# A new instruction order on all engines in the second attention pass of a three-stage kernel

## The chip, the core and the metric

The kernel runs on one core of a Trainium2 chip. The time is that of one execution on the device, in microseconds (us).

## What is computed

Three stages follow one another. The first is a linear attention with a decaying state, for 4 batches of 8 heads, 768 positions and 40 features:

```python
state = np.zeros((B, H, D, D))
for t in range(S):
    kt, vt, rt = (k[:, :, t], v[:, :, t], r[:, :, t])
    wt, at, bt = (w[:, :, t], a[:, :, t], b[:, :, t])
    y[:, :, t] = np.einsum('bhd,bhde->bhe', rt, state)
    Sa = np.einsum('bhde,bhe->bhd', state, at)
    state_decay = state * wt[:, :, None, :] - np.einsum('bhd,bhe->bhde', Sa, bt)
    state = state_decay + np.einsum('bhd,bhe->bhde', vt, kt)
```

The other two are a mixture of 8 experts over the 3072 resulting rows and a dense layer pair. The change touches the attention alone.

## The kernel before, in words

The attention takes the sequence in chunks of 64 positions. There are 24 steps (`STEPS`): 12 chunks for each half of the heads, 16 heads a step. A **first pass** (0 to about 140 us) works out what needs no state: for each step the 64x64 triangular matrix whose inverse couples the positions of a chunk. VectorE inverts two groups of four steps, GpSimd (POOL) the other four groups, and POOL's last inversion ends at 301.6 us, in the second pass. The **second pass** (about 145 to 385 us) carries the state `swt` through the 24 steps. It is what this text is about.

In a step of the second pass TensorE runs 17 batches of 16 small float32 matmuls, each of which is two instructions in the trace (x32). Each batch fills one PSUM bank (`BA` to `BD`), and `done=` names the semaphore `pe_...` (`did[...]`) that it raises. ScalarE or VectorE evicts the bank and raises `ev_...` (`out_of[...]`), for which a later batch waits (`arrive`). All orders are written by hand, one program for each engine. The names:

- `w`, `s`, `ktm`, `u`: batches 2 to 5 of a step, evicted by ScalarE. The trace shows them by operands: `bank<-vtm,g`, `bank<-eye,swt`, `bank<-eye,second`, `bank<-w_tm,inv`.
- `from_s(eye)` (`bank<-eye,st`) and `from_k(vtm)` (`bank<-vtm,ktm`) open the new state in `BD`. They need `ev_s` and `ev_ktm`.
- `z` (`bank<-sa_tm,off`): VectorE adds it to `w_tm`, for which `sa` (the second `bank<-w_tm,inv`) waits.
- `m1` (`bank<-rr,vt`): VectorE masks it (`m<-bank,later`).
- `sa`, `sat`: evicted by ScalarE. `st` closes the new state, and VectorE scales it into `swt`.
- `m2`, `g2` are masked by VectorE. `picks` (`bank<-pick,yt`) works on the rows of the step before. `y` (`bank<-m,btm`) is the last batch, and VectorE's `y_out` (two products into `yt`) evicts its bank `BB` at the start of the next step, before batch 3 (`s`) writes `BB` again.

VectorE also prepares inputs for coming steps. `suffixes(j)` scans `t_in` backward into `suf`, `prefixes(j)` takes a reciprocal and scans forward into `wq`, and `scaled(j)` makes `second` and `alpha`. `gates_of(k)` reduces `picks`' bank into `logit` and needs ScalarE's `rows_of(k)` (`picked<-bank`). On ScalarE `prepare(k)` copies step k's inverses into `inv`. For the first eight steps (`JOINED`) it first patches them with four small copies (line 705).

SyncE's queue (SP) issues nearly all loads, in program order, each behind its waits: `t_in` (776 KB, three slots), `rr`, `vt`, `vtm`, `inv_in`, and `wqx`, the half of `wq` that crosses between partitions. ScalarE issues `ax`, the crossed half of `alpha`. Where a line says L771 it is the helper `heads`, so batches are told apart by operands.

Of the kernel before, what the change touches and what calls it, by code (L numbers as in the profile page):

```python
# [18 lines left out]
C = 64  # L19
# [140 lines left out]
def attention(nc, inp, dram, keep):  # L160

    with ExitStack() as ctx:
# [10 lines left out]
        wqx = ring("wqx", 2, [PARTS, HP, WIDE])  # L173
# [21 lines left out]
        def late_part(n, **sizes):  # L195
# [37 lines left out]
        s_wqx, s_inv_in, s_g1st = ([m_.sem(f"{n}{s}") for s in two] for n in ("s_wqx", "s_inv_in", "s_g1st"))  # L233
# [14 lines left out]
        s_ready, s_choice, s_one = (m_.sem(n) for n in ("s_ready", "s_choice", "s_one"))  # L248
# [21 lines left out]
        def _(sp):  # L270
            def load_t(j):
                if j >= TR:
                    if j - TR < STEPS:
                        sp.wait_ge(s_alpha1, j - TR + 1)
                    elif j - TR == STEPS:
                        sp.wait_ge(s_alpha0, 1)
                    else:
                        sp.wait_ge(s_alpha, j - TR - STEPS)
# [47 lines left out]
            def load_rr(k):  # L326
                if k >= 1:
                    sp.wait_ge(did["m2"], k)
                sp.dma_start(rr[:, :, :], inp["rr"][k]).then_inc(s_vt_rr, 16)

            def load_vtm(k):
                if k >= 1:
                    sp.wait_ge(did["z"], k)
                sp.dma_start(vtm[:, :, :], inp["vtm"][k]).then_inc(s_ax_vtm, 16)
# [70 lines left out]
        def _(dve):  # L405
            dve.memset(keep.ones[:, :], 1.0).then_inc(s_ones, 1)
            dve.memset(keep.eye[:, :], 0.0).then_inc(s_ones, 1)
            dve.memset(restart[:, :, :], 0.0).then_inc(s_set, 1)
            dve.wait_ge(s_set, 1)
            dve.memset(restart[:, :, WIDE - 1:WIDE], 1.0).then_inc(s_set, 1)  # L410
# [5 lines left out]
            dve.wait_ge(s_set, 2)  # L416
# [21 lines left out]
            def prefixes(j):  # L438
                dve.wait_ge(s_suf, j + 1)
                dve.reciprocal(restart[:, :, 0:1], suf[j % 2][:, :, 1:2]).then_inc(s_rw, 1)  # L440
                dve.wait_ge(s_rw, j + 1)
                dve.tensor_tensor_scan(out=forward(wq[j % 3][:, :, :]), data0=forward(w_of(j)), data1=forward(restart[:, :, :]), initial=0.0,
                                       op0=ALU.mult, op1=ALU.add).then_inc(s_wq, 1)
                dve.wait_ge(s_wq, j + 1)
                if j >= STEPS:
                    dve.tensor_copy(wq[j % 3][:, :, WIDE - 1:WIDE], suf[j % 2][:, :, 1:2]).then_inc(s_wc, 1)

            def scaled(j, sem):
                dve.tensor_tensor(second[:, :, :], in_of(j, 1), suf[j % 2][:, :, 2:WIDE], ALU.mult).then_inc(s_second, 1)
                dve.tensor_tensor(alpha[:, :, :], in_of(j, 0), wq[j % 3][:, :, 0:C], ALU.mult).then_inc(sem, 1)  # L450

            def y_out(k):
                dve.wait_ge(did["y"], k + 1)
                dve.wait_ge(s_wqx[k % 2], 32 * turn(k))
                for h, scale in ((0, wq[(STEPS + k) % 3]), (1, wqx[k % 2])):
# [42 lines left out]
            scaled(STEPS, s_alpha0)  # L498
            suffixes(STEPS + 1)
            dve.wait_ge(did["g2"], 1)  # L500
            masked(g2, BC).then_inc(out_of["g2"], 1)
            prefixes(STEPS + 1)
            for k in range(STEPS):
                more = k + 1 < STEPS
                if k >= 1:
                    y_out(k - 1)
                    if k >= 2:
                        gates_of(k - 2)
                    else:
                        dve.sem_inc(out_of["pick"], 1)  # L510
                if k + 2 < STEPS:
                    suffixes(STEPS + k + 2)
                if more:
                    dve.wait_ge(did["ktm"], k + 1)
                    scaled(STEPS + k + 1, s_alpha)
                else:
                    dve.sem_inc(s_alpha, 1)
# [3 lines left out]
                dve.wait_ge(did["m1"], k + 1)  # L521
                masked(m1, BB).then_inc(out_of["m1"], 1)
                if k + 2 < STEPS:
                    prefixes(STEPS + k + 2)
                elif k + 2 == STEPS:
                    dve.wait_ge(s_iota, 8)
                    choices_top(FIRST, chain(dve, s_choice))
                else:
                    dve.memset(one_hot[:, :, FINAL], 0.0)
                    choices_one(FIRST, chain(dve, s_one)).then_inc(s_hot, 1)  # L530
# [3 lines left out]
                else:  # L534
                    dve.wait_ge(s_wqx[(k + 1) % 2], 32 * turn(k + 1))
                    for h, scale in ((0, wq[(STEPS + k + 1) % 3]), (1, wqx[(k + 1) % 2])):
# [10 lines left out]
            link = chain(dve, s_v)  # L547
# [93 lines left out]
        def _(act):  # L641
# [72 lines left out]
            def off_diagonal(k):  # L714
                act.copy(off[:, :, B:C], off_all[:, k])
# [776 lines left out]
```

## Time and profile before

| | |
|---|---|
| median of 3 runs | 1080.39 us (1077.92 to 1081.74) |
| the profiled execution's own time | 1083.37 us |
| its span in the trace | 1081.6 us |
| TensorE busy over the span | 974.9 us (90%) |
| VectorE, ScalarE, POOL busy | 605.9, 316.1, 285.7 us |
| in the second pass, 234.47 to 310.50 us | TensorE 71.43, VectorE 67.46, ScalarE 42.77, POOL 60.69 us busy of 76.03 |
| the same stretch | granted clock 1.00, DMA engines 0.87 busy, 254 GB/s |
| the pass's beginning, 150 to 172 us | granted clock 0.50 |

Busy times of different engines overlap, and a busy share says nothing of which wait ends last. A batch's start in the timeline is when its first matmul starts. "PE" is TensorE, "DVE" VectorE, "ACT" ScalarE, "POOL" GpSimd, and "SPq" is SyncE's DMA queue.

### The profile page before, as it was taken

To read this page: it belongs to the slowest core of one execution; us is meant where nothing else is said; L and a number is where in the kernel's file an instruction comes from. 1 tells how busy PE (TensorE), PEld (TensorE's weight loads), DVE (VectorE), ACT (ScalarE), POOL (GpSimd) and SP (SyncE) were. 2 spreads that over 40 slices of the span, in tenths; PEclk is the share of its full clock that TensorE was granted. 3 is DMA by queue.
4 is the path that set the end of the run, shared out by engine and by line. 5 is a ranking of instruction groups with operands and counts; after the bars stand their busy time and mean duration, and the time that the engine had idled before them with its cause. 6 is when DMAs were issued, how large, how long until landed. Compare 5 with 4: busy or idle time off the path is not lost. (4 is left out here: it accounts for less than half of the span.)

```text
span 1081.6 us, 47466 instructions
## 1 busy us (share of the span) xinstructions
PE 974.9 (90%) x21177; PEld 853.5 (79%) x21178; DVE 605.9 (56%) x981; ACT 316.1 (29%) x737; POOL 285.7 (26%) x351
## 2 busy tenths in 40 slices
PE   3425879999999998999999999979999999999997
PEld 3425769889888866888878888848999999999997
DVE  8896957898988761111211111146656565655655
ACT  5434645655555500011010010031121222222211
POOL 1008989798910003116611100051101000000000
PEclk9999977999999989999999999999999999999999
DMA  6877656998888537996884544320010101010100
GB/s 230 227 176 213 212 162 196 248 262 254 255 248 260 159 116 252 318 307 216 249 274 160 163 160 162 117 79 25 25 25 25 25 1 25 1 25 2 25 1 25
DMA packets 119984, 159.61 MB, mean 148 GB/s; under 512 B 60164, under 2 KB 91028, under 8 KB 119540
## 3 DMA queue, kind: packets, MB, share of 16 engines
q1 hardware_dynamic: 105636, 125.12, 38.5%
q0 software_dynamic: 5824, 25.28, 7.8%
q10 hardware_dynamic: 8464, 8.43, 2.4%
q8 instruction: 36, 0.59, 0.2%
q14 instruction: 24, 0.20, 0.1%
HBM read 133.15 MB, written 19.23 MB: 141 GB/s over the span
## 5 line engine op out<-in xcount | busy, mean ns | idle before, releaser
L1102 DVE TENSOR_SCALAR ht<-h_bank 128x512 f32<-128x512 f32 x62 | 42.8, 691 | 233.4 <-PE h_bank L1079 233.3
L1365 ACT CAST g_hi<-g 128x512 fp32r<-128x512 f32 x96 | 59.6, 620 | 278.6 <-DVE g L1319 278.6
L1090 PE MATMUL y_bank<-w_all,ht 128*128 x496 | 140.4, 437 | 0.3 <-DVE ht L1102 0.3
L1090 PEld LDWEIGHTS y_bank<-w_all,ht 128*128 128x128 f32 x496 | 92.7, 192 | 35.6 <-issue 1.9
L1234 PE MATMUL y_bank<-w_out_hi,g_hi 128*128 128x320 f32 x380 | 118.0, 311 | 1.4 <-DVE g_lo L1299 1.4
L1079 PE MATMUL h_bank<-xt,w 128*128 128x128 f32 x992 | 119.0, 278 | 0.0
L1234 PE MATMUL y_bank<-w_out_hi,g_lo 128*128 128x320 f32 x380 | 117.5, 309 | 0.0
L1234 PE MATMUL y_bank<-w_out_lo,g_hi 128*128 128x320 f32 x380 | 117.3, 309 | 0.0
L1079 PEld LDWEIGHTS h_bank<-xt,w 128*128 128x128 f32 x992 | 113.1, 192 | 3.8
L1221 PE MATMUL h_bank<-xt_hi,w_in_hi 128*128 128x512 f32 x288 | 113.8, 395 | 0.5 <-DVE xt_hi L1282 0.5
L1221 PE MATMUL h_bank<-xt_hi,w_in_lo 128*128 128x512 f32 x288 | 112.6, 391 | 0.0
L1315 DVE TENSOR_SCALAR neg<-h_bank,slope 128x512 f32<-128x512 f32 x96 | 72.0, 750 | 67.1 <-PE h_bank L1221 66.9
L1299 DVE TENSOR_TENSOR g_lo<-g,g_hi 128x512 fp32r<-128x512 f32 x96 | 66.5, 693 | 65.9 <-ACT g_hi L1365 65.9
L127 POOL TENSOR_TENSOR solved<-solved,share 128x31 f32<-128x31 f32 (+15 forms) x124 | 98.3, 793 | 9.7
L771 PE MATMUL bank<-alpha,second 40*64 40x64 f32 x1568 | 45.4, 271 | 59.0 <-DVE alpha L450 57.5
L124 POOL TENSOR_TENSOR share<-solved,blk 128x31 f32<-128x31 f32 (+15 forms) x124 | 91.2, 736 | 9.7
L771 PEld LDWEIGHTS bank<-alpha,second 40*64 40x64 f32 x1568 | 39.2, 180 | 62.0 <-issue 62.0
L95 POOL DMA_INDIRECT x<-x_rows_mid,order x31 | 30.2, 974 | 178.1 <-DVE order L596 101.4
L1234 PEld LDWEIGHTS y_bank<-w_out_hi,g_hi 128*128 128x128 f32 x380 | 71.4, 188 | 6.4 <-DVE g_lo L1299 2.3
L1221 PE MATMUL h_bank<-xt_lo,w_in_hi 128*128 128x512 f32 x192 | 75.3, 392 | 0.0
L1234 PEld LDWEIGHTS y_bank<-w_out_lo,g_hi 128*128 128x128 f32 x380 | 71.4, 188 | 3.1
L1183 POOL DMA_INDIRECT x<-expert_out_mid,position x24 | 25.4, 1057 | 179.4 <-POOLq L979 91.6
(207 smaller groups left out, 1763.4 us busy)
## 6 DMA issues: line engine op xcount, KB each, us to landing
w<-w_in SPq DMA_DIRECT2D x31, 1024.0 KB, 5.9
t_in<-wab_in SPq DMA_DIRECT2D x24, 776.0 KB, 6.2
t_in<-wak_in SPq DMA_DIRECT2D x24, 776.0 KB, 6.7
w_all<-w_in POOLq DMA_DIRECT2D x8, 1280.0 KB, 8.9
rr<-rr_in SPq DMA_DIRECT2D x24, 384.0 KB, 3.3
w_rest<-w_in SPq DMA_DIRECT2D x62, 128.0 KB, 3.1
vt<-vt_in SPq DMA_DIRECT2D x24, 256.0 KB, 3.9
vtm<-vtm_in SPq DMA_DIRECT2D x24, 240.0 KB, 3.4
```

What stands on the lines that cost most here:

```text
L95: pool.indirect_dma_start(out=keep.x[tile % XRING][:, 0:FEAT], out_offset=None, in_=dram["x_rows"], in_offset=bass.IndirectOffsetOnAxis(ap ...
L124: link(eng.tensor_tensor(part, q[:, 0:j + 1, j:j + 1].to_broadcast(shape), h[:, j:j + 1, j + 1:B].to_broadcast(shape), ALU.mult))
L127: link(eng.tensor_tensor(rest, rest, part, ALU.subtract))
L771: last = pe.matmul(out[HALF * to:HALF * to + rows_out, row, n * i:n * i + n], lhs, rhs, start=opens and i == 0, stop=closes and i == HP - 1)
L1079: last = pe.matmul(h_bank[s][h][:, f * ET:(f + 1) * ET], w1[s][:, k, (FH * h + f) * PARTS:(FH * h + f + 1) * PARTS], xt[s][:, k, :], start ...
L1090: last = pe.matmul(y_bank[s][:, 0:FEAT], ht[s][:, f, :], w2[:, ds(e * W2 + f * FEAT, FEAT)], start=f == 0, stop=f == NF - 1)
L1102: dve.tensor_scalar(ht[s][:, FH * n:FH * n + FH, :].rearrange("q f t -> q (f t)"), h_bank[s][n][:, :], 0.0, None, ALU.max).then_inc(s_relu, 1)
L1221: last = pe.matmul(h_bank[j % 2][:, :], w[:, k, f * PARTS:(f + 1) * PARTS], x_part[b % 2][:, k, :], start=n == 0, stop=n == len(passes) - 1)
L1234: last = pe.matmul(y_bank[n][:, 0:FEAT], g_part[j % RING][:, n * PARTS:(n + 1) * PARTS], v[:, f, :], start=f == 0 and p == 0, stop=f == NF ...
L1299: dve.tensor_tensor(g_lo[j % RING][:, :], g[j % 2][:, :], g_hi[j % RING][:, :].bitcast(F32), ALU.subtract).then_inc(s_glo, 1)
L1315: dve.tensor_scalar(neg[j % 2][:, :], h_bank[j % 2][:, :], 0.0, keep.slope[:, f:f + 1], ALU.min, ALU.mult).then_inc(s_neg, 1)
L1365: act.copy(g_hi[j % RING][:, :], g[j % 2][:, :]).then_inc(s_ghi, 1)
```

## The change

On TensorE `m1` moves from behind `z` to right behind `u`, `from_k(vtm)` from ahead of `z` to behind it, and the batch `from_k(m1)` from late in the step to ahead of `sa`. `low_part` (`z`) now reads 64 rows instead of 32. On VectorE `gates_of` goes ahead of `y_out`, `scaled` is split: `alpha` stays early, `second` goes behind the prefix scan, and `m1`'s mask goes ahead of `z`'s sum. The copy of the total into `wq` moves to ScalarE. On ScalarE half of the `off` copy comes early and the other half last. `wqx` gets a third slot. SP's order is new, and `rr` is loaded in two parts.

```diff
@@ SyncE: the loads of a step
             def load_rr(k):
-                if k >= 1:
-                    sp.wait_ge(did["m2"], k)
-                sp.dma_start(rr[:, :, :], inp["rr"][k]).then_inc(s_vt_rr, 16)
+                for part, last in ((slice(HS, HS + HP), "st"), (slice(0, HS), "m2")):
+                    if k >= 1:
+                        sp.wait_ge(did[last], k)
+                    sp.dma_start(rr[:, part, :], inp["rr"][k][:, part, :]).then_inc(s_vt_rr, 16)
...
             for k in range(STEPS):
                 more = k + 1 < STEPS
-                if k + TR < STEPS:
-                    load_t(STEPS + k + TR)
                 if more:
-                    cross_wq(k + 1)
+                    load_vt(k + 1)
+                    load_vtm(k + 1)
+                if k == 0:
+                    load_t(STEPS + TR)
+                    cross_wq(1)
                 if k >= 2:
                     store_rows(k - 2)
                 if more:
-                    load_vtm(k + 1)
-                    load_vt(k + 1)
+                    load_rr(k + 1)
+                if k + TR + 1 < STEPS:
+                    load_t(STEPS + k + TR + 1)
                 if k + 2 < STEPS:
-                    load_inverses(k + 2)
-                if more:
-                    load_rr(k + 1)
+                    cross_wq(k + 2)
                 if k < 2 * GROUP:
                     load_blocks(k + 4 * GROUP)
                 if GROUP < k <= 5 * GROUP:
                     store_inverses(k + GROUP - 1)
+                if k + 2 < STEPS:
+                    load_inverses(k + 2)
@@ ScalarE: a step's end
                 act.copy(by_row(sat[:, :, :]), wide(BA)).then_inc(out_of["sat"], 1)
-                if k + 1 < STEPS:
-                    act.wait_ge(did["z"], k + 1)
-                    off_diagonal(k + 1)
+                if k + 2 < STEPS:
+                    act.wait_ge(s_wq, STEPS + k + 3)
+                    act.copy(wq[(STEPS + k + 2) % 3][:, :, WIDE - 1:WIDE], suf[k % 2][:, :, 1:2]).then_inc(s_wc, 1)
+                if more:
                     prepare(k + 1)
                 if k >= 1:
                     rows_of(k - 1)
+                if more:
+                    off_diagonal(k + 1, 1)
```

**TensorE, inside a step.** Rows from `u` on, first before and then changed. `x15` stands for the rest of a batch of 16.

```order
L771 MATMUL bank<-w_tm,inv 64x40 [waits ev_w]
L771 MATMUL bank<-w_tm,inv 64x40 x15
L771 MATMUL bank<-eye,st 40x40 [waits ev_s,ev_ktm]
L771 MATMUL bank<-eye,st 40x40 x15
L771 MATMUL bank<-vtm,ktm 40x40 x16
L771 MATMUL bank<-sa_tm,off 64x40 [waits ev_u]
L771 MATMUL bank<-sa_tm,off 64x40 x15
L761 REGISTER_ALU
L771 MATMUL bank<-rr,vt 64x64 [waits s_vt_rr]
L771 MATMUL bank<-rr,vt 64x64 x15
L771 MATMUL bank<-w_tm,inv 64x40 [waits ev_z]
L771 MATMUL bank<-w_tm,inv 64x40 x15
```

```order
L803 MATMUL bank<-w_tm,inv 64x40 [waits ev_w]
L803 MATMUL bank<-w_tm,inv 64x40 x15
L803 MATMUL bank<-rr,vt 64x64 [waits ev_s,s_vt_rr]
L803 MATMUL bank<-rr,vt 64x64 x15
L803 MATMUL bank<-eye,st 40x40 [waits ev_ktm]
L803 MATMUL bank<-eye,st 40x40 x15
L803 MATMUL bank<-sa_tm,off 64x40 [waits ev_u]
L803 MATMUL bank<-sa_tm,off 64x40 x15
L803 MATMUL bank<-vtm,ktm 40x40 x16
L803 MATMUL bank<-m,ktm 40x64 [waits ev_m1]
L803 MATMUL bank<-m,ktm 40x64 x15
L803 MATMUL bank<-w_tm,inv 64x40 [waits ev_z]
```

`m1` fills the place in which `from_s(eye)` waited for `ev_ktm`. Between `z` and `sa` there are now two batches where there was one, and between `m1` and the batch that reads it there are three.

**VectorE, a step before up to the state write, and the part of the changed step up to `second`.** `m` is the mask of `m1` or `m2`, `g` that of `g2`.

```order
L456 TENSOR_TENSOR yt<-bank,wq 128x256 [waits s_wqx0,pe_y]
L456 TENSOR_TENSOR yt<-bank,wqx 128x256
L463 TENSOR_REDUCE logit<-bank 128x8 [waits s_rows]
L435 SCALAR_TENSOR_TENSOR suf<-t_in,restart 128x528 [waits s_second,s_t2]
L449 TENSOR_TENSOR second<-t_in,suf 128x512 [waits pe_ktm]
L450 TENSOR_TENSOR alpha<-t_in,wq 128x512
L520 TENSOR_TENSOR w_tm<-w_tm,bank 128x320 [waits pe_z]
L481 TENSOR_TENSOR m<-bank,later 128x512 [waits pe_m1]
L440 RECIPROCAL restart<-suf 128x8 [waits s_suf]
L442 SCALAR_TENSOR_TENSOR wq<-t_in,restart 128x528 [waits s_rw]
L446 COPY wq<-suf 128x8 [waits s_wq]
L537 TENSOR_TENSOR swt<-bank,wq 128x160 [waits s_wqx0,pe_st]
```

```order
L481 TENSOR_REDUCE logit<-bank 128x8 [waits s_rows]
L474 TENSOR_TENSOR yt<-bank,wq 128x256 [waits s_wqx1,pe_y]
L474 TENSOR_TENSOR yt<-bank,wqx 128x256
L439 SCALAR_TENSOR_TENSOR suf<-t_in,restart 128x528 [waits s_second,s_t1]
L468 TENSOR_TENSOR alpha<-t_in,wq 128x512 [waits s_wq,pe_w]
L448 RECIPROCAL restart<-suf 128x8 [waits s_suf]
L499 TENSOR_TENSOR m<-bank,later 128x512 [waits pe_m1]
L543 TENSOR_TENSOR w_tm<-w_tm,bank 128x320 [waits pe_z]
L452 SCALAR_TENSOR_TENSOR wq<-t_in,restart 128x528 [waits s_rw]
L465 TENSOR_TENSOR second<-t_in,suf 128x512 [waits pe_ktm]
```

The reduction into `logit`, which waits for `s_rows`, now stands ahead of the two products into `yt`. `second` has moved from ahead of `alpha` to behind the scan into `wq`.

**SyncE, a step's DMAs, before and changed.** `inv_in` are the inverses and `tt_mid` the solved blocks that are stored.

```order
L280 DMA t_in<-wak_in 128x1552 [waits s_alpha]
L346 DMA wqx<-wq 64x264 [waits ev_y,s_wc]
L346 DMA wqx<-wq 64x264
L350 DMA x_rows_mid<-picked 128x320 [waits s_rows]
L334 DMA vtm<-vtm_in 128x480 [waits pe_z]
L339 DMA vt<-vt_in 128x512 [waits pe_m1]
L324 DMA inv_in<-tt_mid 32x2x128 [waits s_tt0_0,s_ready]
L324 DMA inv_in<-tt_mid 32x2x128 x3
L329 DMA rr<-rr_in 128x768 [waits pe_m2]
L301 DMA tt_mid<-solved 32x32x32
```

```order
L341 DMA vt<-vt_in 128x512 [waits pe_m1]
L336 DMA vtm<-vtm_in 128x480 [waits pe_kv]
L352 DMA x_rows_mid<-picked 128x320 [waits s_rows]
L331 DMA rr<-rr_in 128x256 [waits pe_st]
L331 DMA rr<-rr_in 128x512 [waits pe_m2]
L281 DMA t_in<-wak_in 128x1552 [waits s_second]
L348 DMA wqx<-wq 64x264 [waits ev_y,s_wc]
L348 DMA wqx<-wq 64x264
L302 DMA tt_mid<-solved 32x32x32 [waits s_step]
L325 DMA inv_in<-tt_mid 32x2x128 [waits s_tt2_3,s_ready]
L325 DMA inv_in<-tt_mid 32x2x128 x3
```

The inverse loads have moved from the step's middle, ahead of `rr`, to its very end, behind `t_in` and `wqx`.

## Rows read from the trace of the kernel before

**Rows 1.** Evictions that copy w_tm, one a step: first and last, then step 2.
```profile
L734 ACT COPY w_tm<-bank x24: 426/426/428, 146.4 to 376.7; 128x320 f32<-128x320 f32 x24
...
177.19 0.43 ACT L734 COPY w_tm<-bank 128x320 f32<-128x320 f32 x1 [1.46 <-PE bank L771]
```

**Rows 2.** Timeline of TensorE in one steady step: start us, us, instructions, idle before.
```profile
309.31 0.22 PE L771 MATMUL bank<-swt,alpha 40*64 40x40 f32 x1 [0.29 <-issue]
...
310.23 0.52 PE L771 MATMUL bank<-eye,swt 40*40 40x40 f32 x32
...
311.07 0.68 PE L771 MATMUL bank<-w_tm,inv 64*64 64x40 f32 x32
311.88 0.50 PE L771 MATMUL bank<-eye,st 40*40 40x40 f32 x30
...
312.63 0.67 PE L771 MATMUL bank<-sa_tm,off 32*64 32x40 f32 x32
313.24 0.69 PE L771 MATMUL bank<-rr,vt 40*64 40x64 f32 x32
314.01 0.68 PE L771 MATMUL bank<-w_tm,inv 64*64 64x40 f32 x32
...
315.93 0.69 PE L771 MATMUL bank<-rr,sat 40*64 40x64 f32 x32
...
317.80 0.66 PE L771 MATMUL bank<-m,btm 64*40 64x64 f32 x32
318.75 0.22 PE L771 MATMUL bank<-swt,alpha 40*64 40x40 f32 x1 [0.29 <-issue]
```

**Rows 3.** Timeline of ScalarE, the same step.
```profile
311.31 0.43 ACT L738 COPY ktm<-bank 128x320 f32<-128x320 f32 x1
...
315.20 0.59 ACT L747 COPY sat<-bank 128x512 f32<-128x512 f32 x1
...
318.07 0.43 ACT L727 COPY picked<-bank 128x320 f32<-128x320 f32 x1 [0.44 <-PE bank L833]
```

**Rows 4.** Timeline of VectorE, the same step and the next one's start.
```profile
313.37 0.49 DVE L520 TENSOR_TENSOR w_tm<-w_tm,bank 128x320 f32<-128x320 f32 x1 [0.77 <-PE bank L771]
...
318.52 0.42 DVE L456 TENSOR_TENSOR yt<-bank,wq 128x256 f32<-128x256 f32 x1 [0.55 <-PE bank L771]
318.86 0.41 DVE L456 TENSOR_TENSOR yt<-bank,wqx 128x256 f32<-128x256 f32 x1
```

**Rows 5.** Timeline of ScalarE in a step with patched inverses (step 4).
```profile
200.78 0.59 ACT L747 COPY sat<-bank 128x512 f32<-128x512 f32 x1
...
202.81 1.65 ACT L711 COPY inv<-inv_in 32x256 f32<-32x256 f32 x4
```

**Rows 6.** VectorE by form, 180 to 297 us, then 297 to 377 us.
```profile
L435 DVE TENSOR_TENSOR_SCAN suf<-t_in,restart 128x528 f32<-128x528 f32 x12 | 16.8, 1401 | 0.0
L450 DVE TENSOR_TENSOR alpha<-t_in,wq 128x512 f32<-128x512 f32 x12 | 12.1, 1012 | 0.0
...
L435 DVE TENSOR_TENSOR_SCAN suf<-t_in,restart 128x528 f32<-128x528 f32 x7 | 8.7, 1246 | 0.0
...
L450 DVE TENSOR_TENSOR alpha<-t_in,wq 128x512 f32<-128x512 f32 x8 | 5.5, 685 | 0.0
```

**Rows 7.** Loads of rr, all 24, issue to landing.
```profile
DMA to landing us min/median/max: 2.7/3.3/4.5
```

**Rows 8.** Loads of t_in, all 48, issue to landing.
```profile
DMA to landing us min/median/max: 4.2/6.6/8.7
```

**Rows 9.** Loads of inv_in, all 132, issue to landing.
```profile
DMA to landing us min/median/max: 1.7/2.9/4.7
```

**Rows 10.** SyncE's queue: issue of one step's four inverse loads.
```profile
314.42 1.85 SPq L324 DMA_DIRECT2D inv_in<-tt_mid  x4
```

**Rows 11.** First step of the pass: TensorE's gap, then VectorE's first state write.
```profile
151.62 0.36 PE L771 MATMUL bank<-vtm,ktm 64*40 64x40 f32 x5 [3.06 <-issue]
...
157.53 0.33 DVE L537 TENSOR_TENSOR swt<-bank,wq 128x160 f32<-128x160 f32 x1 [0.87 <-PE bank L771]
```

More of the change, by code:

```diff
@@ L172, in attention @@
         wq = ring("wq", 3, [PARTS, HS, WIDE])
-        wqx = ring("wqx", 2, [PARTS, HP, WIDE])
+        wqx = ring("wqx", 3, [PARTS, HP, WIDE])
         alpha, second = (m_.sb(n, [PARTS, HS, C]) for n in ("alpha", "second"))
@@ L232, in attention @@
         s_t = [m_.sem(f"s_t{s}") for s in range(TR)]
-        s_wqx, s_inv_in, s_g1st = ([m_.sem(f"{n}{s}") for s in two] for n in ("s_wqx", "s_inv_in", "s_g1st"))
+        s_wqx = [m_.sem(f"s_wqx{s}") for s in range(3)]
+        s_inv_in, s_g1st = ([m_.sem(f"{n}{s}") for s in two] for n in ("s_inv_in", "s_g1st"))
         s_blk, s_tt = ([[m_.sem(f"{n}{s}_{part}") for part in range(GROUP)] for s in range(3)] for n in ("s_blk", "s_tt"))
@@ L453, in y_out @@
                 dve.wait_ge(did["y"], k + 1)
-                dve.wait_ge(s_wqx[k % 2], 32 * turn(k))
-                for h, scale in ((0, wq[(STEPS + k) % 3]), (1, wqx[k % 2])):
+                dve.wait_ge(s_wqx[k % 3], 32 * turn(k, 3))
+                for h, scale in ((0, wq[(STEPS + k) % 3]), (1, wqx[k % 3])):
                     last = dve.tensor_tensor(yt[:, HP * h:HP * h + HP, :], BB[:, h, 0:HP * C].rearrange("q (p t) -> q p t", t=C),
@@ L513, in _ @@
                 if more:
[L514 to L517, printed above, removed]
+                    dve.wait_ge(did["w"], k + 1)
+                    dve.wait_ge(s_wq, STEPS + k + 2)
+                    scaled_alpha(STEPS + k + 1, s_alpha)
+                if k + 2 < STEPS:
+                    reciprocals(STEPS + k + 2)
+                dve.wait_ge(did["m1"], k + 1)
+                masked(m1, BB).then_inc(out_of["m1"], 1)
                 dve.wait_ge(did["z"], k + 1)
@@ L534, in _ @@
                 else:
-                    dve.wait_ge(s_wqx[(k + 1) % 2], 32 * turn(k + 1))
-                    for h, scale in ((0, wq[(STEPS + k + 1) % 3]), (1, wqx[(k + 1) % 2])):
+                    dve.wait_ge(s_wqx[(k + 1) % 3], 32 * turn(k + 1, 3))
+                    for h, scale in ((0, wq[(STEPS + k + 1) % 3]), (1, wqx[(k + 1) % 3])):
                         last = dve.tensor_tensor(swt[:, HP * h:HP * h + HP, :], BD[:, h, 0:HP * DIM].rearrange("q (p e) -> q p e", e=DIM),
@@ L712, in prepare, with off_diagonal @@
                 last.then_inc(s_ready, 1)
-            def off_diagonal(k):
-                act.copy(off[:, :, B:C], off_all[:, k])
+            def off_diagonal(k, h):
+                part = slice(HALF * h, HALF * h + B)
+                act.copy(off[part, :, B:C], off_all[part, k])
             def cross_alpha(k):
                 act.wait_ge(s_alpha, k)
-                act.wait_ge(did["w"], k)
                 for h in two:
@@ L729, in _ @@
             act.wait_ge(s_zero, 1)
-            off_diagonal(0)
+            for h in two:
+                off_diagonal(0, h)
             prepare(0)
             for k in range(STEPS):
+                more = k + 1 < STEPS
                 act.wait_ge(did["w"], k + 1)
@@ L753, in _ @@
                     rows_of(k - 1)
+                if more:
+                    off_diagonal(k + 1, 1)
             rows_of(STEPS - 1)
@@ L801, in low_part @@
             def low_part(i, q, m):
-                part = slice(HALF * q, HALF * q + B)
-                return q, q ^ m, C, off[part, slot(q ^ m, i), :], sa_tm[part, slot(q ^ m, i), :]
+                return q, q ^ m, C, off[rows(q), slot(q ^ m, i), :], sa_tm[rows(q), slot(q ^ m, i), :]
             def turned_state(i, q, m):
@@ L947, in _ @@
                 heads(m2_product, BA, C, done="m2")
-                arrive(s_alpha, i)
+                arrive(s_second, i + (STEPS + 1))
                 heads(with_alpha(second), BC, C, done="g2")
-                heads(from_k(lambda i, q, m: m1[rows(m), slot(q, i), :]), BB, C, opens=False, closes=False)
                 arrive(out_of["st"], i + 1)
```

77 lines of the change are left out of this document (46 added, 31 removed).

## The prediction

> **What bounds the kernel now.** I read the page's shares first: TensorE is busy for 90% of the span, but only the second attention pass is changed, and what follows it shifts with its end. Then one row for each step: ScalarE's eviction of `w`. From step 2 (177.19) to step 23 (376.7) there are 21 intervals in 199.5 us, 9.50 us a step [rows 1]. The start is slower, so only steps 2 to 23 are regular.
>
> Next, TensorE's timeline of one step, 309.31 to 318.75, 9.44 us [rows 2]. Batches whose inputs are ready follow at about 0.47 us: `m2`, `g2`, `from_k(m1)` and `picks` take 1.87 us (315.93 to 317.80). The reader should see the intervals that are longer. From `u` to `from_s(eye)` it is 0.81 us (311.07 to 311.88), since ScalarE evicts `ktm` only from 311.31 to 311.74 [rows 3]: 0.35 us lost. From `m1` to `sa` it is 0.77 us (313.24 to 314.01), since VectorE's sum into `w_tm` ends at 313.86 [rows 4]: 0.31 us lost. From `z` to `m1` it is 0.61 us (312.63 to 313.24), 0.15 us too long, whose cause I don't know: a register instruction stands there, and `z` is the only batch on 32-row tiles. The last batch is followed by a loop gap of 0.49 us (317.80 + 0.46 = 318.26, to 318.75). So TensorE is the bound, with some 1.5 us a step in which it computes nothing, half of it waits for evictions.
>
> **TensorE's part of the change.** I count from a step's first matmul, A = 309.31. `u` starts at A + 1.76 and ends at A + 2.22. Now `m1` runs there, to A + 2.68, and `ktm`, evicted by A + 2.43, is ready: 0.35 us saved. `from_s(eye)` (0.34), `z` (0.46) and `from_k(vtm)` (0.41) take it to A + 3.90, `from_k(m1)` to A + 4.36. An engine starts an eviction about 0.27 us after a batch ends (317.80 to 318.07 [rows 2, 3]), and TensorE goes on 0.15 us after an eviction (313.86 to 314.01 [rows 2, 4]). VectorE masks `m1` from A + 2.95 to A + 3.64, sums `z` from A + 3.76 to A + 4.25, and `sa` may start at A + 4.40, 0.04 us after its place: 0.31 us saved nearly whole. The wait of `m2` for `sat` is untouched. A step would be 9.44 - 0.35 - 0.31 = 8.78 us, or 8.63 if the 0.15 us go as well. I take **8.70 us**.
>
> **What VectorE asks.** While POOL works, `suf` takes 1.40 us instead of 1.25 and `alpha` 1.01 instead of 0.69 [rows 6], together 0.48 us. Both now lie ahead of `m1`'s mask. After `y_out` (until A + 0.79), `suf`, `alpha` and the reciprocal reach A + 2.8 in the quiet case, 0.15 us before `m1` is ready; with POOL they reach A + 3.25, the mask ends at A + 3.95, and `from_k(m1)` starts at A + 4.10 instead of 3.90. With the few hundredths that `z` adds, or hides, I take 0.15 us: **8.85 us** with POOL. `second` is covered: `g2` needs it more than two batches later than before. Moving the total's copy to ScalarE frees VectorE and costs ScalarE less than the 0.43 us of the far larger `picked` copy [rows 3].
>
> **What ScalarE asks, and `gates_of` ahead of `y_out`.** This is the added wait. `y_out` now queues behind the reduction into `logit`, which waits for `rows_of`, which ScalarE does after `prepare`. `s` needs `BB` free at A' + 0.92 of the next step (309.31 to 310.23 [rows 2]). In an ordinary step, with S the start of the `sat` eviction, the next step begins at S + 3.10 now: `m2` at S + 0.73 (315.20 to 315.93 [rows 2, 3]), four batches to S + 2.61, gap 0.49. `picks` ends at S + 2.15, `rows_of` runs from 2.42 to 2.85, that is to A' - 0.25. With 0.15 us and 0.13 for the reduction, `y_out` starts at A' + 0.03 and takes 0.34 + 0.41 [rows 4]; `s` may start at A' + 0.93. It just fits.
>
> In the steps with patched inverses it does not. There ScalarE came to its inverse copies at 202.81 and was through at 204.46, S + 3.68 for S = 200.78 [rows 5]. The `off` copy ahead of them goes and the total's small copy comes. I take the sum of both 0.1 us shorter (0.1 us either way is 0.6 us in six steps), S + 3.58, and `rows_of` ends at S + 4.01 = A' + 0.91. Then `y_out` starts at A' + 1.19, ends at 1.94, and `s` starts at 2.09 instead of 0.92: 1.17 us late. ScalarE's and VectorE's later work has that much more room, so nothing is added. These six steps (2 to 7: `gates_of` starts at step 2, and `prepare` patches up to inverse 7) take 8.70 + 1.15 = **9.85 us**.
>
> **The loads.** In the steady order each load keeps some room. `m2` ends at A + 6.8, so the second part of `rr` goes out at A + 7.1, and `m1` needs it at A' + 2.22 = A + 10.9: 3.8 us against 3.3 in the median and 4.5 at most for the whole of `rr` [rows 7]. Behind it come `t_in`, `wqx`, the stored blocks, and the four inverse loads, which take 1.85 us to issue [rows 10], from about A + 9.5 to 11.4. The last lands after 2.9 us [rows 9] at about A + 13.9, and `prepare` wants it at A + 15.0. I price the loads at nothing; the cover that hides them is 1.1 us for the inverses and 0.5 for `rr`.
>
> In the first step alone `wqx` for the next state write goes out behind `from_k(vtm)` and a `t_in`, where it was issued before the loop's work. That step has a 3.06 us gap of TensorE that ends at 151.62, and the state write was at 157.53 [rows 11]. I put the `wqx` issue at 155 to 156. If it lands as quickly as the fastest small load (1.7 us [rows 9]) nothing is lost. If it lands only behind the `t_in` issued at about 154, after 6.6 us [rows 8], the write is 2.6 to 3 us late, of which TensorE sees about 1.2, since two more batches stand ahead of `picks`. I take **+1.0 us**, nearer the second end.
>
> The Trainium skill (DMA: Bandwidth & Descriptors, Queues, rings and completion order) says that descriptors are consumed in ring order on each DMA engine. By that rule a small load behind `t_in` is served after it, and the sum would keep the 1.2 us; no row before shows `wqx`'s landing.
>
> **The sum.** Before, 22 steps (2 to 23) of 9.50 us are 209.0 us. Now 6 x 9.85 + 7 x 8.85 (steps 8 to 14, until POOL ends near 300 us) + 9 x 8.70 = 59.1 + 62.0 + 78.3 = 199.4 us: -9.6. With +1.0 it is -8.6 us. The profiled execution took 1083.37 us and would take 1074.8. The median of the runs is 1080.39, so the forecast is **1072 us**.
>
> **Rivals.**
> 1. The patched steps cost nothing: `rows_of` comes early enough, or VectorE's wait is shorter than I make it. Then 6 x 1.15 = 6.9 us more are gained: 1065 us. For it speaks that ScalarE is idle for long stretches; against it the chain of [rows 5].
> 2. The saved waits are partly taken over. `sa` has 0.04 us too little and `s` 0.01 us, so any slower eviction, or POOL's full slowing of VectorE, counts at once. With 0.3 us more in each of 16 ordinary steps: 1072 + 4.8 = 1077 us.
> 3. TensorE's clock comes back later. It stands at 1.2 GHz, half of full, from 150 to 172 us. The first two steps took 30.8 us (146.4 to 177.19 [rows 1]) against 19.0 for two regular ones, so the gap and the 22 us at the low level cost 11.8 us, some 8.7 of them the clock (11.8 less the 3.06 us gap), 0.4 us for each us. A stall in the first step may shift the return: 5 to 12 us more at the low level make it 1074 to 1077 us.
> 4. The other side: the inverse loads, now last in line, come late. Against 1.1 us of room, a landing of 4.7 us [rows 9] is 0.6 late. `t_in`, ahead of them, lands after up to 8.7 us [rows 8] instead of 6.6, at A + 16.1; inverses served behind it come 1.1 to 1.5 us late. `prepare` then delays `rows_of`, the reduction, `y_out` and `s` one for one. The 16 ordinary steps turn the gain into a loss above 8.6 / 16 = 0.54 us each; at 1.2 us it is 1072 + 19 = 1091 us. Against it: SyncE's wait list and the landings of before show loads well ahead of their users. The Trainium skill's rule of ring order (same page and section) would favour this rival whenever `t_in` is slow.
>
> **Numbers.** The forecast has 0.58, rival 1 0.14, rivals 2 and 3 together 0.20, rival 4 0.08. The range 1065 to 1079 holds the first three but for their tails. No change is what a measurement can't tell from it, 0.3% or 3.2 us, so faster means below 1077.2. Forecast and rival 1 lie there nearly whole, rivals 2 and 3 for more than half: faster 0.84, same 0.09, slower 0.07.
>
> **What would show it.** In the changed profile `w` evictions should be 9.8 to 9.9 us apart in steps 2 to 7, about 8.85 to step 14, and 8.7 after it. `from_s(eye)` and `sa` should follow without a gap. In steps 2 to 7 TensorE should pause ahead of `bank<-eye,swt` for over 1 us, with `yt` as the releaser, behind a `logit` reduction that waits for `picked`. The first `swt` write should wait for `wqx`. I am wrong if the first eight steps are as quick as the others, if TensorE waits for `vt_rr` or `inv` appears late, or if the low clock lasts beyond 175 us.

## The result, and the profile of the changed kernel

The changed kernel is slower: 1086.59 us in the median of 9 runs (1083.67 to 1091.98) against 1080.39 us (9 runs on the same chip), a ratio of 1.006 (95% interval 1.0032 to 1.0088). I had forecast 1072 us. Its profiled span is 1083.9 us.

The evictions of `w`, one a step, answer to [rows 1]: the row for all 24, and those of steps 2 to 4.

```profile
L761 ACT COPY w_tm<-bank x24: 426/426/428, 144.9 to 381.1; 128x320 f32<-128x320 f32 x24
...
173.18 0.43 ACT L761 COPY w_tm<-bank 128x320 f32<-128x320 f32 x1
183.05 0.43 ACT L761 COPY w_tm<-bank 128x320 f32<-128x320 f32 x1
192.73 0.43 ACT L761 COPY w_tm<-bank 128x320 f32<-128x320 f32 x1
```

From step 2 to step 23 it is now 207.9 us where it was 199.5. The 21 intervals, read from the same evictions, are 9.87, 9.68, 9.67, 12.94, 12.85, 10.03, 12.04, 10.20, then 8.82, 8.83, 9.03, 8.81, 9.26, 9.81, 12.49, and then five of 8.81 to 8.85 and one of 9.37. So three kinds of step stand side by side: ordinary ones of 8.8 us and patched ones of 9.7 to 9.9 us, both near the forecast, and six of 10 to 13 us (steps 5 to 9 and 16) that nothing in my sum contains; 9.26, 9.81 and 9.37 lie between.

An ordinary step of TensorE, beside [rows 2] (start, us, instructions):

```profile
268.08 0.22 PE L803 MATMUL bank<-swt,alpha 40*64 40x40 f32 x1 [0.19 <-issue]
...
269.85 0.68 PE L803 MATMUL bank<-w_tm,inv 64*64 64x40 f32 x32
270.33 0.69 PE L803 MATMUL bank<-rr,vt 40*64 40x64 f32 x32
270.82 0.51 PE L803 MATMUL bank<-eye,st 40*40 40x40 f32 x32
271.16 0.68 PE L803 MATMUL bank<-sa_tm,off 64*64 64x40 f32 x32
271.62 0.52 PE L803 MATMUL bank<-vtm,ktm 64*40 64x40 f32 x32
271.97 0.77 PE L803 MATMUL bank<-m,ktm 64*40 64x64 f32 x32
272.53 0.68 PE L803 MATMUL bank<-w_tm,inv 64*64 64x40 f32 x32
...
275.40 0.68 PE L864 MATMUL bank<-pick,yt 40*64 40x48 f32 x32
276.04 0.66 PE L803 MATMUL bank<-m,btm 64*40 64x64 f32 x32
276.92 0.22 PE L803 MATMUL bank<-swt,alpha 40*64 40x40 f32 x1 [0.22 <-issue]
```

`from_s(eye)` follows `m1` after 0.49 us and `z` is 0.46 us long instead of 0.61: the three gaps of before are closed. Two small ones are new: `from_k(m1)` to `sa` takes 0.56 us, and `picks` to `y` 0.64 instead of 0.47. Start to start it is 8.84 us.

The long steps, by windows from one `w` to the next (us, busy time of each engine with its instructions, granted clock, DMA share, GB/s): steps 2 to 4, 5, 6, and 10 to 14.

```profile
173.18:202.40 29.22, 26.33 (x1728) 25.07 (x1728) 24.38 (x43) 21.63 (x58) 23.65 (x39) 1.00 0.93 240
202.40:215.34 12.94, 9.55 (x576) 9.06 (x576) 8.27 (x15) 7.32 (x20) 11.61 (x18) 0.92 1.04 248
215.34:228.19 12.85, 11.91 (x576) 11.54 (x576) 8.81 (x15) 7.21 (x20) 11.75 (x15) 0.68 0.59 134
...
260.46:305.21 44.75, 43.25 (x2888) 41.61 (x2880) 41.33 (x70) 30.09 (x76) 40.91 (x50) 1.00 0.93 266
```

In step 5 TensorE is idle for 3.4 of 12.94 us while the DMA engines are full. In step 6 it is busy for 11.91 of 12.85 us with the same batches: the granted clock is 0.68. By windows of 1 us it fell to half of full (1.2 of 2.4 GHz) near 213.3 us, behind two idle gaps of 0.55 and 1.64 us, and was full again near 223.6. A late load is paid twice here.

What step 5 waits for: SyncE's queue from the end of step 4 on, then ScalarE, then TensorE's batches with a wait.

```profile
201.61 0.53 SPq L295 DMA_DIRECT2D blk<-g_mid  x1
202.24 2.57 SPq L325 DMA_DIRECT2D inv_in<-tt_mid  x4
...
206.19 0.35 SPq L336 DMA_DIRECT2D vtm<-vtm_in  x1
...
209.90 0.43 SPq L281 DMA_DIRECT2D t_in<-wak_in  x1
210.43 1.11 SPq L348 DMA_DIRECT2D wqx<-wq  x2
211.58 0.60 SPq L295 DMA_DIRECT2D blk<-g_mid  x1
212.23 0.86 SPq L302 DMA_DIRECT2D tt_mid<-solved  x1
213.18 5.57 SPq L325 DMA_DIRECT2D inv_in<-tt_mid  x4
```

```profile
208.18 0.21 ACT L779 COPY wq<-suf 128x8 f32<-128x8 f32 x1
211.56 1.22 ACT L730 COPY inv_in<-late 16x128 f32<-16x128 f32 x4 [3.17 <-DMA inv_in<-tt_mid]
212.81 1.64 ACT L736 COPY inv<-inv_in 32x256 f32<-32x256 f32 x4
214.47 0.43 ACT L752 COPY picked<-bank 128x320 f32<-128x320 f32 x1
```

```profile
213.03 0.22 PE L803 MATMUL bank<-swt,alpha 40*64 40x40 f32 x1 [1.64 <-DMA vtm<-vtm_in]
215.97 0.77 PE L803 MATMUL bank<-eye,swt 40*40 40x40 f32 x32 [1.18 <-DVE yt L474]
```

ScalarE waits 3.17 us for the inverses; `rows_of` is late by that, the reduction and `y_out` behind it, and TensorE stands ahead of `s` (`bank<-eye,swt`). The inverses that it waits for are those sent from 202.24 us on, right behind `blk`. All four were out by 204.81, and the wait ended at 211.56, some 7 us after the last of them went out, where a landing took 2.9 us in the median before [rows 9]. The `vtm` for which TensorE waits went out at 206.19 and took 6.6 us to land, against 3.4 us in the median before. So step 5 loses its time to landings, and not to the 5.57 us of issue: this begins at 213.18, when both waits are over. The block load ahead of those inverses landed after 9.1 us. Landings of `blk` from 185 to 260 us, in the kernel before, in the changed one and in inv_ahead_small (see below):

```profile
DMA to landing us min/median/max: 3.5/3.8/4.4
DMA to landing us min/median/max: 4.8/6.4/9.1
DMA to landing us min/median/max: 3.2/4.0/4.9
```

The Trainium skill (DMA: Bandwidth & Descriptors, Queues, rings and completion order) says that each DMA engine takes its descriptors in ring order, the rule by which rival 4 was to be feared. The trace agrees for the blocks: `blk` landed at 210.74, and the wait for the inverses sent behind it ended at 211.56. (`vt`, sent later still, had landed at 210.61, so landings don't come strictly in the order of issue.)

The long issue is a second loss, and it shows in steps 7 and 8. The four inverse loads behind `blk` and `tt_mid` again take 5.55 us to issue where they had taken 1.85 [rows 10], 4.11 us of it the first of them. SyncE sends `vt` and `vtm` only behind them, and TensorE stands for 2.45 us, though `vtm` lands after 3.2:

```profile
237.08 1.45 SPq L295 DMA_DIRECT2D blk<-g_mid  x1
238.58 0.88 SPq L302 DMA_DIRECT2D tt_mid<-solved  x1
239.55 5.55 SPq L325 DMA_DIRECT2D inv_in<-tt_mid  x4
245.15 0.42 SPq L341 DMA_DIRECT2D vt<-vt_in  x1
245.62 0.43 SPq L336 DMA_DIRECT2D vtm<-vtm_in  x1
249.06 0.22 PE L803 MATMUL bank<-swt,alpha 40*64 40x40 f32 x1 [2.45 <-DMA vtm<-vtm_in]
```

The waits of TensorE over the pass (us in total, times, longest):

```profile
PE bank L803 <- DVE yt L474: 5.9, 9, 1.2
PE bank L803 <- DMA vtm<-vtm_in: 5.4, 4, 2.4
PE bank L803 <- DMA rr<-rr_in: 0.8, 1, 0.8
```

### The profile page after: what moved, and what is told of

Same layout as the page of the kernel before. It is cut to its first block and busy times, and to the rows that moved or that the text cites. A ratio compares the mean times of both kernels' runs of the same rounds, so it can differ in the third digit from the quotient of the medians.

```text
span 1083.9 us, 47514 instructions
## 1 busy us (share of the span) xinstructions
PE 973.4 (90%) x21177; PEld 855.6 (79%) x21178; DVE 600.0 (55%) x959; ACT 331.6 (31%) x783; POOL 282.6 (26%) x351
## 5 line engine op out<-in xcount | busy, mean ns | idle before, releaser
L127 POOL TENSOR_TENSOR solved<-solved,share 128x31 f32<-128x31 f32 (+15 forms) x124 | 94.0, 758 | 9.7
L124 POOL TENSOR_TENSOR share<-solved,blk 128x31 f32<-128x31 f32 (+15 forms) x124 | 94.0, 758 | 9.7
L1265 PEld LDWEIGHTS y_bank<-w_out_hi,g_lo 128*128 128x128 f32 x380 | 71.3, 188 | 0.0
```

What stands on the lines that cost most here:

```text
L124: link(eng.tensor_tensor(part, q[:, 0:j + 1, j:j + 1].to_broadcast(shape), h[:, j:j + 1, j + 1:B].to_broadcast(shape), ALU.mult))
L127: link(eng.tensor_tensor(rest, rest, part, ALU.subtract))
L1265: last = pe.matmul(y_bank[n][:, 0:FEAT], g_part[j % RING][:, n * PARTS:(n + 1) * PARTS], v[:, f, :], start=f == 0 and p == 0, stop=f == NF ...
```

## The experiments

Runs on different chips differ by up to 0.6% in the kernel before, so a ratio to it, on its own chip, is what is compared. "Intervals" is the time from step 2's `w` eviction to step 23's in the one profiled execution (199.5 us before, 207.9 changed); the stages behind the pass vary by some us from one execution to the next, and this figure leaves them out. Where a kernel's results are wrong, its text says what it leaves out.

| kernel | ratio to before (95%) | intervals, us |
|---|---|---|
| after_again | 1.0075 (1.0042 to 1.0109) | 207.0 |
| inv_mid | 1.0014 (0.9973 to 1.0055) | 206.4 |
| sp_before | 0.9978 (0.9944 to 1.0012) | 199.1 |
| yout_first | 0.9993 (0.9953 to 1.0032) | 199.6 |
| before_inv_last | 1.0024 (0.9981 to 1.0067) | 200.8 |
| less_t | 0.9933 (0.9898 to 0.9968) | 197.2 |
| before_less_t | 0.9999 (0.9969 to 1.0029) | 199.5 |
| rr_whole | 1.0016 (0.9982 to 1.0049) | 199.4 |
| sp_before_whole_yout | 0.9961 (0.9936 to 0.9985) | 193.5 |
| less_t_yout | 0.9910 (0.9873 to 0.9947) | 191.7 |
| wqx_first | 0.9894 (0.9854 to 0.9934) | 192.2 |
| wqx_first_gates | 0.9923 (0.9899 to 0.9946) | 195.0 |
| wqx_first_inv_last | 0.9984 (0.9952 to 1.0016) | 201.4 |
| wqx_first_split | 0.9864 (0.9821 to 0.9907) | 189.3 |
| inv_ahead_small | 0.9947 (0.9922 to 0.9972) | 194.2 |

**inv_mid**, the inverse loads in their old place.

```diff
                     store_rows(k - 2)
+                if k + 2 < STEPS:
+                    load_inverses(k + 2)
                 if more:
                     load_rr(k + 1)
...
-                if k + 2 < STEPS:
-                    load_inverses(k + 2)
```

> The changed kernel with one edit: SyncE issues a step's four inverse loads where the kernel before has them, ahead of rr, instead of last behind t_in, wqx, the blocks and the stores. Theory A (the inverse loads' place in line is what costs): the steps of 12 to 13 us in the changed profile go, ScalarE's waits for inv_in with them, steps 8 to 22 take 8.8 to 8.9 us, steps 2 to 7 still 9.7 to 9.9, and the time is 1070 to 1075 us. Theory B (at less than 9 us a step the DMA engines are simply full, whatever the order): the late loads show up elsewhere, at vtm or rr, several steps stay above 10 us, and the time stays at 1083 to 1088 us.

ScalarE's waits for inverses went, and TensorE's for `rr`, now behind them, came (one row, the waits of TensorE):

```profile
PE bank L803 <- DMA rr<-rr_in: 11.3, 10, 2.4
```

Seven steps stood above 10 us, at other places than in the changed kernel. This is the picture of theory B, late loads that show up elsewhere, though the ratio of 1.0014 is a little better than its time. By itself the old place is no cure. That `m1`, three batches earlier than before, has no 2 us to give to `rr` is not the whole reason: in sp_before and wqx_first the inverse loads stand ahead of `rr` too, and TensorE waits for `rr` for only 0.4 and 1.5 us. What in the rest of SyncE's order makes the difference is open.

**sp_before**, SyncE's loop as before.

```diff
             for k in range(STEPS):
                 more = k + 1 < STEPS
+                if k + TR < STEPS:
+                    load_t(STEPS + k + TR)
                 if more:
-                    load_vt(k + 1)
-                    load_vtm(k + 1)
...
```

> The changed kernel with SyncE's whole loop order as in the kernel before (t_in and wqx first, inverses in the middle, rr behind them, blocks and stores last; rr still in two parts). Theory A (order in line): 1070 to 1075 us like the kernel with the inverse loads alone moved back, and a first state write that waits less for wqx. If t_in a step sooner or rr ahead matters by itself, this is slower than that kernel by 2 us or more. Theory B (DMA engines full): 1083 to 1088 us.

It had one wait for `rr` (0.4 us) and nine for `wqx` (8.5 us). The gain of theory A (0.6% and more) did not come, nor theory B's 1083 us: the loss was gone, the gain was not there.

**yout_first**, VectorE's `y_out` ahead of the reduction.

```diff
+                if k >= 1:
+                    y_out(k - 1)
                 if k >= 2:
                     gates_of(k - 2)
                 elif k == 1:
                     dve.sem_inc(out_of["pick"], 1)
-                if k >= 1:
-                    y_out(k - 1)
```

> The changed kernel with VectorE's y_out ahead of gates_of again, as before. Theory A says that late inverse loads delay rows_of, and that this reaches TensorE only because y_out queues behind the reduction: with y_out first a late load still delays inv, but steps 2 to 4 fall from 9.7 to about 8.9 us, and the total falls by 4 to 8 us, to 1079 to 1083 us. A rival: the long steps start from loads that TensorE itself waits for (vtm, rr), so that they stay, and the gain is only that of steps 2 to 4, 2 to 3 us.

Steps 2 and 3 took 8.80 and 9.26 us, but steps 6 to 9 still 11.4 to 12.5, behind waits for `inv_in` and `vtm` (6.7 us of TensorE for `vtm`). The total fell by 0.7 to 0.8 points, as theory A had it, and the long steps stayed, as the rival had it.

**before_inv_last**, the kernel before with the inverse loads last.

```diff
-                if k + 2 < STEPS:
-                    load_inverses(k + 2)
                 if more:
                     load_rr(k + 1)
...
                     store_inverses(k + GROUP - 1)
+                if k + 2 < STEPS:
+                    load_inverses(k + 2)
```

> The kernel before with one edit: the four inverse loads last in SyncE's line, as in the changed kernel. Theory A in its strong form (the place alone costs): ScalarE waits for inverses, and it is 3 to 8 us slower than the kernel before, 1083 to 1088 us. If instead the place costs only together with the shorter step and y_out behind the reduction: within 2 us of the kernel before, 1079 to 1082 us.

Nearly nothing, within an interval that still allows 0.7%: a step of 9.45 us has room for the late place. No wait for an inverse load stands in its profile, although the issue took 2.87 to 3.55 us in steps 5 to 7, where blocks and stored inverses both go out right ahead.

**less_t and before_less_t**, less traffic. Both leave out the 256 KB a step from which `second` is made, so their results are wrong.

```diff
-                sp.dma_start(t_in[j % TR][:, :], src).then_inc(s_t[j % TR], 16)
+                n = W_COLS + (2 if j < STEPS + TR else 1) * A_COLS
+                sp.dma_start(t_in[j % TR][:, 0:n], src[:, 0:n]).then_inc(s_t[j % TR], 16)
```

> The changed kernel, its order untouched, with less traffic: from step 3 of the second pass on, t_in's loads leave out the part from which second is made (256 of 776 KB; second is then computed from stale data, so its results are wrong). Theory B (the DMA engines are nearly full once steps take less than 9 us, so that some load is late in any order): the long steps go, the waits for vtm, rr and inv_in with them, the clock stays up, and the time is 1068 to 1075 us. Theory A (only the place of the inverse loads in line): they still stand last, behind t_in, the blocks and the stores, and most long steps stay, 1080 us or more.

> The kernel before with the same 256 KB less in each t_in load of the second pass from step 3 on (wrong results in the same way). Its steps of 9.45 us wait for no load, so both theories expect no change: within 2 us of the kernel before. If it gains as much as the changed kernel does, less traffic helps by something else than the late loads.

The changed kernel gained, the kernel before did not: what it lost was time on the queues. Steps 8 and 9 stayed long, 11.2 us each, at a lower clock behind waits for `vtm`. As a ratio 0.9933 lies where theory B had it (1068 to 1075 us on the chip of the result). The profiled execution of less_t took 1088.87 us against a median of 1078.44, so its step times are weaker evidence than the ratio. In it the inverse loads still took 4.3 to 5.2 us to issue in the steps with both blocks and stores ahead. So less traffic takes most of the loss away with the order untouched: order and load of the queues act together.

**rr_whole**, `rr` in one DMA.

```diff
-                for part, last in ((slice(HS, HS + HP), "st"), (slice(0, HS), "m2")):
-                    if k >= 1:
-                        sp.wait_ge(did[last], k)
-                    sp.dma_start(rr[:, part, :], inp["rr"][k][:, part, :]).then_inc(s_vt_rr, 16)
+                if k >= 1:
+                    sp.wait_ge(did["m2"], k)
+                sp.dma_start(rr[:, :, :], inp["rr"][k]).then_inc(s_vt_rr, 16)
```

> The changed kernel with rr loaded in one DMA behind m2, as before, instead of in two parts. Theory B counts packets too: the split makes 128 packets more a step and cuts 3 KB rows to 1 and 2 KB; with one DMA the engines have a little less to do, but rr goes out whole behind m2 and lands 0.3 to 0.6 us later. It expects 1080 to 1088 us, no clear change. If the split is what fills the queues, the long steps go and the time is 1075 us or less.

Its profile was milder than the changed kernel's two; the interval leaves open whether that is the edit.

**sp_before_whole_yout** joins three of these edits.

> The changed kernel's engine orders with SyncE's loop as before, rr in one DMA and y_out ahead of gates_of: the pieces that should leave the gain and take the losses away. Theory B (every order has some late load while steps are short, the order of before the fewest) expects steps 2 to 7 at 8.9 to 9.3 us, a few steps above 9.5, and 1072 to 1077 us. A rival: rr in one DMA comes too late for m1, which is now two batches earlier, and the time is 1078 us or more.

Its median was 1080.74 us, but on a chip on which the kernel before took 1086.24; by the ratio of 0.9961 it lies in theory B's range. Steps 2 to 7 took 8.90 to 9.54 us, TensorE waited for `rr` for 1.1 us only, and VectorE's state writes waited for `wqx` ten times, 7.5 us in all.

**after_again, less_t_yout and wqx_first.** The first is the changed kernel unedited, the second joins less_t and yout_first, the third is sp_before_whole_yout with this:

```diff
+                if more:
+                    cross_wq(k + 1)
                 if k + TR < STEPS:
                     load_t(STEPS + k + TR)
-                if more:
-                    cross_wq(k + 1)
```

> The changed kernel itself, unedited, beside the next two on one chip. If the loads that come late differ from one execution to the next, its profile shows long steps of over 9.9 us at other steps than the first one did (which had steps 5, 6, 7, 8, 9 and 15), each behind a wait for inv_in, vtm or rr, and the clock lower after the larger ones. If they come from the place of each load in the program alone, it is the same steps. Time: 0.2 to 0.9% slower than the kernel before.

> The changed kernel with both suspected causes away: t_in's loads 256 KB lighter from step 3 of the second pass on (second is then computed from stale data, so its results are wrong) and y_out ahead of gates_of. If the short step is worth what the prediction said and the two causes are all that took it back, steps 2 to 22 take 8.8 to 9.0 us with one or two exceptions, the 21 intervals from step 2 to step 23 together 186 to 191 us (199.5 in the kernel before), and the time is 0.9 to 1.3% below the kernel before. If something else costs, steps stay at 9.5 us or more.

> The kernel with SyncE's loop as before, rr in one DMA and y_out first, and one more edit: wqx goes out ahead of t_in at the head of a step instead of behind it. That kernel's state writes waited ten times for wqx, 7.5 us together. If the place behind t_in makes wqx late, these waits go, the 21 intervals from step 2 to 23 fall from 193.5 us to 187 to 190, and the time is 0.6 to 1.0% below the kernel before. If t_in, sent 1.1 us later, or another load takes over, the intervals stay above 192 us.

The changed kernel had its long steps at 5 to 9 again (11.1, 11.1, 11.1, 12.9, 12.7 us), and none of 12 us at 16: most of it is fixed by the program. With both causes away (less_t_yout) one step of 12.0 us was left, and the intervals came to 191.7 us, 0.7 above the range expected. In wqx_first the ten waits for `wqx` were gone, the ordinary steps took 8.9 us, and it was 1.1% below the kernel before, where 0.6 to 1.0% was expected; but the intervals, 192.2 us, fell by only 1.3 us, with five waits for `vtm` (3.2 us) in their place:

```profile
L757 ACT COPY w_tm<-bank x24: 425/425/427, 144.2 to 363.8; 128x320 f32<-128x320 f32 x24
...
171.60 0.42 ACT L757 COPY w_tm<-bank 128x320 f32<-128x320 f32 x1
```

**wqx_first_gates, wqx_first_inv_last and wqx_first_split** each put one piece of the change back into wqx_first: the reduction ahead of `y_out`, the inverse loads last, and `rr` in two parts. Their edits are those of yout_first, before_inv_last and rr_whole, the first and the last read backward.

> The fast kernel wqx_first with one edit back: gates_of ahead of y_out, as in the changed kernel. If the reduction's place costs by itself what the prediction said, steps 2 to 7 take 9.7 to 9.9 us instead of 8.97 to 9.93 and the ordinary steps stay at 8.9: the time is 3 to 6 us above wqx_first, 0.5 to 0.8% below the kernel before. If its price comes mostly from carrying late inverse loads over to TensorE, there is nothing to carry here, and it is within 2 us of wqx_first.

> wqx_first with the inverse loads last in SyncE's line, as in the changed kernel. If this place costs by itself, steps 5 to 9 (blocks and stores go out right ahead) take over 10.5 us, ScalarE waits for inv_in, and it is 5 us or more above wqx_first. If it costs only with y_out behind the reduction, ScalarE's waits for inv_in show but the steps stay below 10 us, and the time is within 3 us of wqx_first.

> wqx_first with rr in two DMAs, as in the changed kernel. If the 128 packets more a step load the queues, waits for vtm or wqx come back, several steps stand above 9.3 us, and it is 2 to 5 us slower than wqx_first. If the early first part of rr is what helps, TensorE's waits for rr (1.5 us in five places) go and it is 1 to 2 us faster.

With the reduction first, steps 2 to 7 took 9.72 to 9.82 us but for one of 10.28 late in that stretch, and the intervals grew by 2.8 us. With the inverse loads last it was some 9 us more, yet ScalarE waited for none. They took up to 3.90 us to issue, most in steps 5 to 7, and the next `vtm`, behind them in the queue, came late in 16 steps (waits of TensorE):

```profile
PE bank L799 <- DMA vtm<-vtm_in: 12.4, 16, 1.8
```

The split of `rr` costs nothing; its kernel is the fastest of all, at 0.9864, though its interval overlaps that of wqx_first.

**inv_ahead_small**, one edit in the changed kernel: the inverse loads move past two DMAs.

```diff
                     cross_wq(k + 2)
+                if k + 2 < STEPS:
+                    load_inverses(k + 2)
                 if k < 2 * GROUP:
                     load_blocks(k + 4 * GROUP)
                 if GROUP < k <= 5 * GROUP:
                     store_inverses(k + GROUP - 1)
-                if k + 2 < STEPS:
-                    load_inverses(k + 2)
```

> The changed kernel with the inverse loads behind t_in and wqx but ahead of the blocks and the stored inverses, whose rows are 128 bytes. If these two are what holds the inverse loads up in steps 5 to 9, the waits for inv_in there go, their issue takes 2 to 3 us instead of up to 5.6, steps 5 to 9 fall from 11 to 13 us to below 10.5, and it is 0 to 0.3% slower than the kernel before. If t_in ahead of them is enough, nothing changes: 0.5 to 0.8% slower.

SyncE's queue of this kernel in the corresponding steps, and ScalarE's waits for inverses over the pass:

```profile
213.26 0.43 SPq L281 DMA_DIRECT2D t_in<-wak_in  x1
213.79 1.11 SPq L348 DMA_DIRECT2D wqx<-wq  x2
215.00 1.99 SPq L325 DMA_DIRECT2D inv_in<-tt_mid  x4
217.03 0.42 SPq L295 DMA_DIRECT2D blk<-g_mid  x1
217.50 0.56 SPq L302 DMA_DIRECT2D tt_mid<-solved  x1
```

```profile
ACT inv L736 <- DMA inv_in<-tt_mid: 1.6, 3, 0.8
```

The issue is back at 1.99 us. Steps 2 to 8 took 9.62 to 9.73 us, one 10.84, the ordinary ones 8.81. It does better than I expected: 0.5% faster than the kernel before, where the changed kernel is 0.6 to 0.75% slower.

## Why the prediction was wrong, by its steps

**TensorE's part: right.** 8.70 us an ordinary step was forecast, and 8.81 to 8.85 came. The 0.35, 0.31 and 0.15 us are gone. The sum missed two new gaps, 0.10 us before `sa` and 0.17 before `y`, which now waits for `m2`'s mask.

**POOL's slowing of VectorE: hidden.** I had 8.85 us for steps with POOL, and steps 10 to 13 of the changed kernel took 8.82, 8.83, 9.03 and 8.81, hardly more than the 8.81 to 8.85 behind POOL's end.

**The reduction ahead of `y_out`: the step length right, the price too high.** The chain from [rows 5] gave 9.85 us for steps 2 to 7; the quiet ones took 9.67 to 9.87, and 9.62 to 9.73 in inv_ahead_small. My price was 1.15 us in each of six steps, 6.9 us. In wqx_first_gates the edit by itself cost 2.8 us of the intervals, because steps 2 to 7 of wqx_first take 8.97 to 9.93 us without it. It has a second price that I named only within rival 4: it carries any lateness of ScalarE over to TensorE.

**The first steps: mis-sized.** I took +1.0 us. From the first `w` to step 2's it is 28.3 us (144.88 to 173.18) against 30.8: 2.5 us were gained, though the state write did wait 4.7 us for `wqx` in one place. The low clock and a gap with no releaser take most of these two steps in every kernel, and such gaps fell elsewhere in each profile.

**"I price the loads at nothing; the cover that hides them is 1.1 us for the inverses and 0.5 for `rr`" is the step that failed.** Its working took both the 1.85 us of issue and the 2.9 us of landing from a kernel in which the inverse loads stood in the middle of the line and a step took 9.45 us. The landing failed first: behind a block load that landed after 9.1 us, the inverses of step 4 landed some 7 us after the last of them went out, and ScalarE waited 3.17 us. The issue failed next: where blocks and stored inverses both go out right ahead (steps 5 to 7) it took 4.2 to 5.6 us, and `vt` and `vtm` of the next step stood behind it. A room of 1.1 us covers neither. inv_ahead_small shows that it was the place directly behind those two DMAs, not the place behind `t_in` or `wqx`: moving past them changes the ratio from 1.006 and 1.0075 to 0.9947, and the intervals from 207.9 and 207.0 to 194.2 us. That is 13 us, more than the whole forecast gain. Less traffic does much the same with the order left alone (less_t), so the place costs this much only together with this much traffic. In inv_ahead_small the intervals are 3.5 us above my sum for them (6 x 9.85 + 7 x 8.85 + 8 x 8.70 = 190.7).

**Rival 4 had the mechanism, at a chance of 0.08, and the wrong spread.** I spread it over 16 ordinary steps at 0.5 to 1.2 us each, from `t_in`'s slowest landing. In truth most of it strikes steps 5 to 9 in both profiles of the changed kernel, at up to 4 us. Blocks alone (steps 0 to 4) or stores alone (8 to 20) go out in many steps of ordinary length; both together go out in steps 5 to 7, and steps 8 and 9 trail them. Only step 16 of the first profile is long outside this stretch, behind a wait of 1.85 us of ScalarE and 0.75 us of TensorE in step 15. And the clock multiplies it: step 6 took 3.2 us more than a quiet patched step of 9.67 us at a granted clock of 0.68, with a wait of 1.18 us of its own. I had looked at the clock only in the pass's first steps, and had `t_in` as the load that makes the inverses late; with `t_in` still ahead of them in inv_ahead_small ScalarE waits for them for 1.6 us in all.

That the engine orders are worth about what I said of them is shown by wqx_first and wqx_first_split: 1.1 and 1.4% faster than the kernel before. My 0.8% contains the reduction's price, which these two don't pay; without it my sum gives 1065 us, 1.4%.

Left open: why four loads take 5.6 us to issue behind those two DMAs and 2 us ahead of them. The profile shows the duration and not what SyncE's queue waits for. Nor does a run tell the two DMAs apart, or their 128-byte rows from their size. Whether `rr` in one part changes anything is open too: rr_whole and wqx_first_split point in opposite directions, within their intervals.

## What to carry to other kernels

When a step gets shorter, the DMA queue is the same length: price each load's place anew, by what stands directly ahead of it, and count its issue time as well as its landing. Here two transfers in rows of 128 bytes stood in front of urgent loads, and it paid to put them behind; that the rows are the reason is a guess. And a wait that was harmless may become dear by what queues behind it: put the work that another engine waits for (`y_out`) ahead of work that waits for a third (the reduction).

## What the runs showed of the hardware that was not expected

In the middle of a pass that was otherwise at 90% busy the granted clock fell to half behind idle gaps of TensorE of 0.55 and 1.64 us (step 5), of 2.45 us (step 8) and of 0.75 and 0.83 us (steps 15 and 16), and one step then took 12.85 us with 11.91 busy. A gap of 1.59 us in after_again, at 233.08 us, left it at full, so the length of one gap does not decide. In the kernel before, the 0.5 us of a step of 9.45 in which TensorE is not busy never lowered it after step 2. The duration of a DMA's issue on SyncE's queue is not fixed: four inverse loads took 1.85, 1.99, 3.90 and 5.57 us in different orders of the same transfers. Nor is the landing: a block load of 128 KB landed after 3.8 us in the median before and after 6.4 us, 9.1 at most, in the changed kernel.
